# Turning the rows and columns of two mixers by VectorE's 32x32 block transposes and transfers between partitions, instead of by TensorE

## The reference

```python
def _attn_ref(q, k, v, n_global, n_local):        # B, H, S, D = 2, 8, 768, 64
    scores = matmul(q, k.T) / sqrt(D) + bias       # bias: -slope[h] * distance
    a = softmax(where(is_global | is_local, scores, -1e9))   # 8 global keys, 96 local ones
    return matmul(a, v)

def _moe_ref(x, w_tok1, w_tok2, w_ch1, w_ch2):     # x: (2, 768, 512)
    h = relu(x.T @ w_tok1) @ w_tok2                # across tokens, 768 -> 256 -> 768
    u = x + h.T
    return u + relu(u @ w_ch1) @ w_ch2             # across channels, 512 -> 1536 -> 512

def _moe2_ref(x, w_theta, w_tok_r, w_tok_i, w_ch):
    theta = x @ w_theta
    zr, zi = x * cos(theta), x * sin(theta)
    u = x + w_tok_r @ zr + w_tok_i @ zi            # across tokens
    return u + relu(u @ w_ch)
```

## Time and profile before

| | us |
|---|---|
| median of 3 runs | 513.64 (513.61 to 514.79) |
| the profiled execution | 514.9 |
| its span, first to last instruction | 512.7 |
| PE busy in the span | 504.5 |
| DVE busy | 258.8 |
| ACT busy | 173.9 |
| POOL busy | 144.2 |

### The profile page before, as it was taken

The page is one execution under the profiler, slowest core; times in us unless marked ns, Lnnn a source line. Parts: engine busy times, 40 slices in busy tenths (PEclk is TensorE's granted clock), DMA queues, the critical chain, the costliest instruction groups (busy, mean ns, idle before and its releaser), DMA issues.

```text
span 512.7 us, 8107 instructions
## 1 busy us (share of the span) xinstructions
PE 504.5 (98%) x3049; PEld 471.1 (92%) x3049; DVE 258.8 (50%) x679; ACT 173.9 (34%) x371; POOL 144.2 (28%) x143
## 2 busy tenths in 40 slices
PE   7999999999999999999999999999999999999997
PEld 5899999879999999979999999998888899888897
DVE  7999998552111421164111424166775565754452
ACT  6899898521111111122111143413322320321130
POOL 4576766199900000005000041820310310000040
PEclk9999999999999999999999999999999999999999
DMA  5886675135410000003000011420000011000002
GB/s 195 310 301 233 221 264 160 45 123 150 137 42 1 0 2 0 1 0 99 28 0 1 0 63 61 124 83 0 1 1 2 0 63 61 1 1 0 1 31 93
DMA packets 9112, 37.20 MB, mean 73 GB/s; under 512 B 1136, under 2 KB 3184, under 8 KB 7664
## 3 DMA queue, kind: packets, MB, share of 16 engines
q1 hardware_dynamic: 9072, 36.67, 21.1%
HBM read 33.52 MB, written 3.15 MB: 72 GB/s over the span
## 4 chain that ended last, share of the span: by engine, by line
PE 91%; DMA 3%; DVE 2%; issue 1%; POOL 1%; ACT 1%; DVEq 0%; POOLq 0%; ACTq 0%
PE bank L272 72%; PE bank L1360 7%; PE bank L1125 3%; PE bank L1155 3%; PE bank L1158 2%; DMA qk_raw<-qk 2%; PE bank L1139 1%; PE bank L1137 1%; PE bank L1216 1%; PE bank L1243 1%; POOL wsplit L506 1%; DMA counts<-both_counts 1%; PE bank L1165 0%; DVE scores L903 0%; ACT bias L618 0%
## 5 line engine op out<-in xcount | busy, mean ns | idle before, releaser
L272 PE MATMUL bank<-hid,wsplit 128*128 128x384 f32 (+1 forms) x648 | 126.4, 344 | 0.1
L272 PEld LDWEIGHTS bank<-hid,wsplit 128*128 128x128 f32 x648 | 113.2, 188 | 4.0 <-issue 0.7
L272 PE MATMUL bank<-split,wsplit 128*128 128x384 f32 x576 | 108.1, 337 | 0.0
L272 PE MATMUL bank<-wsplit,zs 128*128 128x512 f32 (+1 forms) x576 | 104.1, 340 | 0.0
L272 PEld LDWEIGHTS bank<-wsplit,zs 128*128 128x128 f32 x576 | 89.1, 188 | 13.3
L272 PEld LDWEIGHTS bank<-split,wsplit 128*128 128x128 f32 x576 | 100.3, 188 | 0.0
L1034 DVE SCALAR_TENSOR_TENSOR hid<-bank,hid 128x384 fp32r<-128x384 f32 x48 | 26.7, 557 | 140.4 <-ACT hid L732 140.4
L574 POOL TENSOR_TENSOR wsplit<-wraw,wsplit 128x1536 fp32r<-128x1536 f32 (+1 forms) x18 | 58.7, 3263 | 75.5 <-ACT wsplit L693 74.5
L732 ACT ACTIVATE hid<-bank 128x384 fp32r<-128x384 f32 x48 | 23.6, 491 | 143.4 <-PE bank L272 143.4
L573 POOL CAST wsplit<-wraw 128x1536 fp32r<-128x1536 f32 (+1 forms) x12 | 15.9, 1328 | 136.1 <-PE bank L272 122.8
L506 POOL TENSOR_TENSOR wsplit<-qk_raw,wsplit 64x256 fp32r<-64x256 f32 x48 | 38.9, 810 | 26.5 <-DVE wsplit L810 24.8
(11 more groups left out here) (101 smaller groups left out, 583.3 us busy)
## 6 DMA issues: line engine op xcount, KB each, us to landing
wraw<-weights SPq DMA_DIRECT2D x16, 768.0 KB, 4.2
qk_raw<-qk SPq DMA_DIRECT2D x11, 1056.0 KB, 5.5
vt<-v SPq DMA_DIRECT2D x10, 520.0 KB, 5.2
out<-act_raw SPq DMA_DIRECT2D x16, 192.0 KB, 1.9
wraw<-weights SPq DMA_DIRECT2D x4, 512.0 KB, 3.5
qk_raw<-qk SPq DMA_DIRECT2D x2, 264.0 KB, 3.5
qk_raw<-qk SPq DMA_DIRECT2D x1, 528.0 KB, 6.0
vt<-v SPq DMA_DIRECT2D x2, 260.0 KB, 6.4
```

The lines of the kernel that those rows point to most:

```text
L272: mm = pe.matmul(dst, lhs(a), rhs(c), start=first and i == 0, stop=last and i == 2, skip_group_check=True)
```

## The change

PE makes no transposes in the mixers any more. A full turn of 128x128 is made of two steps: DVE turns every 32x32 block in place (`dve.transpose`), and SP moves the blocks between the groups of 32 partitions, 16 transfers at a time (`move_quads`). The turned `x` lies in a new tile `xT`, 32 columns at a time.

The first mixer now adds in the turned layout. `x` is turned before it is needed: for batch 0 in attention (DVE, steps 26, 29, ..., 41), for batch 1 beside `hidden` of batch 0. `mixed_tokens(i, j)` has its operands exchanged: `h1` is loaded as the weights and `w_tok2` streams, so that `h` comes out with channels on the partitions, 384 tokens (half `c`, block `k_`) at a time, in the banks of `U_BANK`. DVE adds it to `xT` in place. ACT's `hi` and DVE's `lo` are then both made from `xT`, in SBUF. In the second mixer `multiply_x` reads the turned rows from `xT`, which DVE's transposes beside `hidden` of batch 1 and beside the last two `mix` of batch 0 prepare.

```diff
+        def move_quads(sp, src, first, count, done):
+            from_ = src.rearrange("p (t q c) -> p t q c", t=count, q=P // QUAD)
+            to = xT[:, first * DM:(first + count) * DM].rearrange("p (t a c) -> p t a c", t=count, a=P // QUAD)
+            for a in range(P // QUAD):
+                for q in range(P // QUAD):
+                    sp.dma_start(to[q * QUAD:(q + 1) * QUAD, :, a],
+                                 from_[a * QUAD:(a + 1) * QUAD, :, q]).then_inc(done, 16)
+
+        def turn_rows(dve, dst, b, t):
+            return dve.transpose(dst, act_raw[:, b, t * DM:(t + 1) * DM].rearrange(
+                "p (k q i) -> p q k i", k=KD, q=P // QUAD))
...
@@ sync
+            sp.wait_ge(x_turned, T)
+            move_quads(sp, turned_early[:, :], 0, T, xT_in)
             general_sync(sp, load_flag(sp))
             for i in range(len(BESIDE), len(ORDER)):
                 load_weight(i)
+                if i == SLOTS + 1:
+                    for first in range(0, T, STAGED):
+                        sp.wait_ge(x_turned, T + first + STAGED)
+                        move_quads(sp, turned[:, :], first, STAGED, xT_in)
+                if i == SLOTS + 3:
+                    for first in range(0, T, STAGED):
+                        sp.wait_ge(x_turned, 2 * T + first + STAGED)
+                        move_quads(sp, turned[:, :], first, STAGED, x_rows_in)
...
@@ gpsimd
                 if i == len(BESIDE):
                     pool.wait_ge(pv_done, STEPS)
                     pool.wait_ge(tile_lo, T)
+                    pool.wait_ge(xT_in, BATCH_IN)
                 if i == SLOTS + THETA:
-                    pool.wait_ge(h_ready, B * T)
+                    pool.wait_ge(h_ready, B * OUTB)
@@ scalar
-                for s in range(T):
-                    act.wait_ge(uT_ready, b * T + s + 1)
...
+                for i in range(OUTB):
+                    act.wait_ge(u_done, b * OUTB + i + 1)
...
+                    act.activation(by_quads(split[:, 0, u_cols(i)]), xT_at(i), ACT.Copy).then_inc(uT_hi, 1)
@@ vector, attention
+                t, off = divmod(m - TURN_FROM, TURN_EVERY)
+                if 0 <= t < T and off == 0:
+                    dve.wait_ge(x_done, 2 * t + 2)
+                    turn_rows(dve, turned_early[:, t * DM:(t + 1) * DM], 0, t).then_inc(x_turned, 1)
@@ vector, multiply_x
-                x_rows = bank[7 if g else 5][:, :]
+                t = g % T
+                x_rows = xT[:, t * DM:(t + 1) * DM].rearrange("p (a k j) -> p k a j", a=P // QUAD, k=KD)
@@ vector, first mixer
+                def lo_of_u(i):
+                    dve.wait_ge(uT_hi, b * OUTB + i + 1)
+                    dve.tensor_tensor(by_quads(lo_[:, u_cols(i)]), xT_at(i),
+                                      by_quads(hi[:, u_cols(i)].bitcast(F32)), ALU.subtract).then_inc(uT_lo, 1)
+
+                dve.wait_ge(xT_in, (2 * b + 1) * BATCH_IN)
+                for i in range(OUTB):
+                    dve.wait_ge(h_ready, b * OUTB + i + 1)
+                    dve.tensor_tensor(xT_at(i), by_quads(U_BANK[i][:, 0:SC]), xT_at(i),
                                       ALU.add).then_inc(u_done, 1)
+                    if i:
+                        lo_of_u(i - 1)
+                lo_of_u(OUTB - 1)
@@ tensor, angles
-                for d in range(KD):
-                    mm = pe.transpose(bank[7 if g else 5][:, d * P:(d + 1) * P],
-                                      act_raw[:, b, d * S + s * P:d * S + (s + 1) * P], ident[:, :])
-                mm.then_inc(xr_ready, 1)
@@ tensor, first mixer
+                def mixed_tokens(i, j):
+                    c, k_ = divmod(i, KD)
                     pe.wait_ge(h1_lo, b * KJ + j + 1)
...
+                    return three(pe, U_BANK[i][:, 0:SC], lambda a: h1s[:, j, a, k_ * P:(k_ + 1) * P],
+                                 lambda a: w_at(TOK2, a, j * S + c * SC, SC), j == 0, j == KJ - 1)
+
+                for i in range(KD):
+                    mixed_tokens(i, 0)
+                for i in range(KD):
+                    mixed_tokens(i, 1).then_inc(h_ready, 1)
+                for i in range(KD, OUTB):
+                    mixed_tokens(i, 0)
+                    mixed_tokens(i, 1).then_inc(h_ready, 1)
...
@@ tensor, hidden and reduce_hidden
-                    if f == 0:
-                        pe.wait_ge(uT_lo, b * T + (c + 1) * T // NC)
+                        pe.wait_ge(uT_lo, b * OUTB + (c + 1) * KD)
```

More of the change, by code:

```diff
@@ L71 @@
 HALF = 1024
+QUAD = 32
+TURN_FROM = 26
+TURN_EVERY = 3
+STAGED = 3
+BATCH_IN = 16 * 16
 BORROWED = 5
@@ L162, in build @@
         zc = sb("zc", [P, DM])
-        u_rows = sb("u_rows", [P, 2, DM], F32, mix1_mem)
+        turned = sb("turned", [P, STAGED * DM], F32, mix1_mem)
         hid = sb("hid", [P, 2 * 3 * SC], F32R, mix1_mem)
@@ L218, in build @@
         u_done = sem("u_done")
-        uT_ready = sem("uT_ready")
+        x_turned = sem("x_turned")
+        xT_in = sem("xT_in")
+        gen_turned = sem("gen_turned")
+        gen_xT = sem("gen_xT")
         uT_hi = sem("uT_hi")
@@ L398, in general_vector @@
                 dve.wait_ge(gen_x, B * H * T + 1)
+                dve.wait_ge(xT_in, BATCH_IN)
+                for t in range(T):
+                    turn_rows(dve, turned_early[:, t * DM:(t + 1) * DM], 0, t).then_inc(gen_turned, 1)
+                dve.wait_ge(gen_xT, BATCH_IN)
                 for g in range(AHEAD):
@@ L460, in _ @@
                 load_weight(i)
+                if i == SLOTS + 1:
[6 more added lines that the diff above has]
+                        move_quads(sp, turned[:, :], first, STAGED, x_rows_in)
+            for first in range(0, T, STAGED):
+                sp.wait_ge(x_turned, 3 * T + first + STAGED)
+                sp.wait_ge(prod_done, 2 * (first + STAGED))
+                sp.wait_ge(x_rows_in, (T + first) // STAGED * BATCH_IN)
+                move_quads(sp, wraw[:, first // STAGED, 0:STAGED * DM], first, STAGED, x_rows_in)
             for j in range(B * OUTB):
@@ L1069, in _ @@
                         tile_to_lo(B * T + g + 2)
+                    if b == 0 and s >= T - 2:
+                        dve.wait_ge(w_ready, len(ORDER))
+                        dve.wait_ge(x2_done, B * NC * KD)
+                        for t in range(STAGED):
+                            half = s - (T - 2)
+                            turn_columns(dve, wraw[:, half, t * DM:(t + 1) * DM], 1,
+                                         half * STAGED + t).then_inc(x_turned, 1)
                 def add_y(d, off, n, src, col):
@@ L1235, in _ @@
                     wait_weight(TOK2)
-                def turn_u(s):
-                    g = b * T + s
-                    pe.wait_ge(u_done, g + 1)
-                    if g >= 2:
-                        pe.wait_ge(uT_lo, g - 1)
-                    for d in range(KD):
-                        mm = pe.transpose(bank[4 + s % 2][:, d * P:(d + 1) * P],
-                                          u_rows[:, s % 2, d * P:(d + 1) * P], ident[:, :])
-                    mm.then_inc(uT_ready, 1)
-                def mixed_tokens(s, j):
-                    g = b * T + s
-                    pe.wait_ge(h1_lo, b * KJ + j + 1)
-                    if j == 0 and s >= 4:
-                        pe.wait_ge(u_done, g - 3)
-                    if b and j == 0 and s < 4:
-                        pe.wait_ge(acc_taken, ((b * NC) - 1) * KD + s + 1)
-                    return three(pe, bank[s % 4][:, :], lambda a: w_at(TOK2, a, j * S + s * P, P),
-                                 lambda a: h1s[:, j, a], j == 0, j == KJ - 1)
@@ L1288, in reduce_hidden @@
                     pe.wait_ge(r1_lo, g + 1)
+                    if i == 0:
+                        pe.wait_ge(u_done, (b + 1) * OUTB)
                     for d in range(KD):
```

83 lines of the change are left out of this document (48 added, 35 removed).

## The result

The changed kernel takes 521.0 us (median of 4 runs, 519.25 to 521.32), the kernel before in the same job 514.21 us (513.61 to 514.9). The ratio is 1.012, with an interval of 1.0099 to 1.0141: slower by 6.8 us, where I had forecast 520.8 us. The profiled execution after took 519.25 us, the fastest of its four; its span is 517.5 us, that of before 512.7 us.

A forecast was written before the change was run, and what follows sets the result against it. TensorE, busy 504.5 of 512.7 us, was taken as the bound. -6.5 - 4.2 + 14.15 + 1.0 + 0.8 + 2.0 = +7.2 us gave 520.8 us against the runs' median; own case 517.5 to 524, 8 in 10 from 513 to 526.

The forecast's parts named there:

- main step: First mixer, batch 0: each of eight two-SBUF-input `lo` on DVE waits out one POOL instruction, 20 us plus 2 us.
- rival without holding: `lo_of_u` runs at its own 0.55 us beside POOL; 503.7 us, faster; chance 0.10.
- TensorE's spared time in the first mixer: First product to first `reduce_hidden`: 12.49 us without waits instead of 15.74; 3.25 us a batch, 6.5 us in all.
- Stall of batch 0: TensorE waits for held `lo` in two pieces; `reduce_hidden(0)` at 130.1 instead of 115.95, 14.15 us.
- Batch 1: Only the last two `lo` meet POOL; `reduce_hidden(0)` 13.5 us after the first product instead of 12.5, 1.0 us.
- Second mixer: TensorE spared 12 groups of four transposes at 0.35 us each, 4.2 us.
- Attention: Six 128x512 transposes among DVE's steps 26 to 41, 0.61 us each, 3.6 us, of which 0.8 us taken as cost.
- estimate of 1.24 us: Attention: by the Trainium skill's 311 ns per 128x128 transpose, four take 1.24 us; the term would be about 4 us.
- Pace after the second stall: TensorE's matmuls restart slowly after idling in batch 0; bounds 0 and 2.1 us, taken as 2.0 us.
- Transfers: Sixteen SP issues a batch at 0.33 us, 8 us a batch, nothing on the path; 17 us available in the first.

The follow-up runs named there:

- e1_psum: Changed kernel, but DVE writes `u` back into its PSUM bank and `hi` and `lo` are made from the bank: 506.4 us, ratio to before 0.984.
- e2_gate: Changed kernel, but POOL's second weight chunk after attention waits until the eight `lo` of batch 0 are done: 510.77 us, ratio to before 0.993.
- e7_held_before: Kernel before, but its `lo_of_uT` reads `act_raw` in SBUF in place of the bank, so two SBUF inputs: 522.68 us, ratio to before 1.0146.
- e5_rows_pe: e1_psum with the 48 transposes of `act_raw` back on TensorE, without DVE's column transposes and their transfers: 511.75 us, ratio to before 0.994.
- e6_double: e1_psum with each of the six transposes in attention done twice: 510.31 us, ratio to before 0.992.
- e3_fill: Changed kernel with 14 unused 512-column matmuls on TensorE between `hidden(1)` and `reduce_hidden(0)` of batch 0: 519.44 us, ratio to before 1.0086.
- e4_thirds: Changed kernel, but POOL splits each of the eight chunks after attention in three pieces of 512 columns: 513.09 us, ratio to before 0.997.
- e10_four: e1_psum with four extra 128-column matmuls ahead of the first `reduce_hidden` of each batch, results unused: 505.93 us, ratio to before 0.983.

## Why the prediction was right

Its main step, eight `lo` at one POOL instruction each, held in detail. I had the fourth end at 118.7 and `hidden(0)` start there; it ended at 118.26 and `hidden(0)` started at 118.40. I had `reduce_hidden(0)` at 130.1; it came at 129.76. e1_psum removes the cause and with it 14.6 us (my rival without holding, 503.7 us, is this kernel to within 2.7 us); e2_gate removes it from POOL's side; e7_held_before puts the cause alone into the kernel before and reproduces a slowdown. That my 520.8 us met the median of 521.0 us to 0.2 us is luck: the terms below are off in both directions, and the profiled spans differ by 4.8 us where my sum has 7.2. What remained of the other steps:

- TensorE's spared time in the first mixer, 3.25 us a batch: e1_psum has 12.80 and 12.82 us against 15.74, so 2.9 a batch. The rest is the 2.12 pace and 0.2 us in the 48 products.
- Stall of batch 0, 14.15 us: 26.44 - 12.49 = 13.95.
- Batch 1, 1.0 us: 249.63 - 235.71 = 13.92 us, so 1.4 over the 12.5. The last two `lo` are held, as said, in TensorE's records a wait of 0.93 us:

```profile
235.71 8.75 PE L285 MATMUL bank<-wsplit,hid 128*128 128x384 f32 x48
...
249.63 2.35 PE L285 MATMUL bank<-hid,wsplit 128*128 128x384 f32 x12 [0.93 <-DVE hid L1102]
```

- Second mixer, 4.2 us: 12 x (11.71 - 11.28) = 5.2, where 11.71 is the distance of two theta blocks in the kernel before (350.10 to 361.81); e5_rows_pe confirms it in time, with 5.3. I had taken the distance of two rows within a block, 0.35 us, as the price of four transposes; the distance from block to block shows 0.43. The 48 matmuls behind the transposes take 8.56 us there to the next row and 8.48 without them, so a part of the price falls behind the group.
- Attention, 0.8 us: the profile after shows nothing (first product 103.32 and 103.46 before), the profiles together 0 to 1.3 us. The price of one transpose, 0.61 us apart, was right (0.63), and the estimate of 1.24 us that stood beside it is twice too dear; that an additional one is on the path is shown only beyond the six (e6_double).
- Pace after the second stall, 2.0 us: 3.66 - 2.08 = 1.6; e3_fill shows it as a cost of its own. That the row I took it from is of the same kind is not shown: over the 5.16 us of the earlier trace rows the granted clock reads 1.00, here 0.56. So that the size came near may be luck.
- Transfers, nothing on the path: right, though an issue holds SP for 0.69 us (11.09 us for 16), twice my 0.33. Weights are loaded from 95.43 instead of 83.79, and POOL still starts at 100.62. A load takes 4.0 us to land, so some 1 us was to spare, not the 17 us less 8 that I had counted with; in e4_thirds the same queue did cost time.

In sum, of the two profiled spans: batch 0 +10.7, its pace +1.6, batch 1 -1.8 (13.92 for 15.75), second mixer -5.2, attention -0.1: +5.2 us, measured +4.8. My sum was +7.2. I mis-sized two terms most, second mixer and attention, and both to the disadvantage of the change, 2 us together. The medians differ by 6.8 us because the profiled execution after is 1.75 us under its median and that of before 0.7 us above. Why executions of the changed kernel spread over 2 us isn't shown. Part may be the clock: its mean over the span is 0.987 in the three slower ones and 0.990 in the profiled one; an estimate from these is 3 us more at half speed, 1.5 us lost. But e3_fill spreads over 2 us at 0.993 alike.

## What to carry to other kernels

Before work moves to VectorE, look at where both inputs of each of its operations will lie, and whether GpSimd is running there: one input in PSUM makes the difference between 0.55 and up to 3.6 us, and here between 8 us faster and 7 us slower with the same work taken off TensorE. Where the holding can't be avoided, cut GpSimd's instructions short, and then check every queue that its later end pushes back. Price a small group on TensorE by the distance between the same point in two whole periods, not by its own rows.

## What the hardware showed that I had not expected

- The holding goes one for one. Beside POOL's unbroken run in batch 0 (the changed kernel, e3_fill, e7_held_before) DVE's next operation with two SBUF inputs came through after a single POOL instruction each time, and POOL's after a single `lo`; POOL loses 0.3 to 0.5 us a cast by it.
- TensorE has two steady paces for the same 384-column matmuls at full granted clock: 2.08 and 2.12 us per 12, kept for up to 45 groups, about 3 us over e1_psum's two batches. It differs between kernels, and in e10_four, e2_gate and e7_held_before between the batches of one kernel. What chooses it is open.
- Behind an idle of 3.18 us (e2_gate) the granted clock was 0.55 over the next twelve matmuls, 3.76 us instead of 2.08; behind one of 0.80 us (e7_held_before) and one of 1.99 us (e3_fill) it was 1.00 (2.19 and 2.18 us).
- Issuing a transfer between partitions (32 partitions, in pieces of 512 bytes) holds SP for 0.69 us, where a load from outside holds it for 0.33 us.
